# Decayed keys by token: one GpSimd product with a table, two chunks ahead, in place of TensorE transposes and a ScalarE copy

## The chip, the core and the metric

The kernel runs on one core of a Trainium2 chip, as one program. The metric is the device time of one execution in microseconds (us). The engines are named as in the profile: PE (TensorE), PEld (its weight loads), DVE (VectorE), ACT (ScalarE), POOL (GpSimd) and SP (SyncE, which here only starts transfers).

## The reference

Three layers follow each other on 2 sequences of 768 tokens with 384 features. Only the first is touched by the change:

```python
def _attn_ref(r, k, v, w, u):            # B=2, H=8, S=768, D=48
    state = np.zeros((B, H, D, D))
    for t in range(S):
        kt, vt, rt = (k[:, :, t], v[:, :, t], r[:, :, t])
        cur = np.einsum('bhd,bhe->bhde', u[None] * kt, vt)
        y[:, :, t] = np.einsum('bhd,bhde->bhe', rt, state + cur)
        state = w[None, :, :, None] * state + np.einsum('bhd,bhe->bhde', kt, vt)
    return y
```

The second is a mixture of experts: each token takes one of 8 experts by its logits, or that of the token before it, goes through `relu(x @ w1[e]) @ w2[e]`, and is scaled by its probability. The third is a gated MLP with a product across the 768 tokens. Inputs and outputs are float32.

## The kernel before

The attention layer is the first stage of the program and takes about its first 87 us. Its 768 x 2 tokens are cut into 12 chunks of 128 tokens (`NC = 12`), six to a sequence (`NCB = 6`). The loop over tokens becomes products of matrices per chunk, with powers of the decay `w` folded into r and k. All engines run their own list of instructions in order, each in a loop over the chunk number n, and they meet only at semaphores. For one chunk n:

- DVE, `decay(n)` (lines 635 and 636): `k_dec` is k by feature times the table `tab_k`, and `r_dec` is r by feature times `tab_r`. Each is 128 x 512.
- PE, `scores_of(n)` (line 1095): 8 products of `k_dec` and `r_dec`; DVE, `mask(n)` (line 643) keeps the causal half.
- PE, `keysT_of(n)` (line 1108): 4 transposes bring `k_dec` to the layout by token in bank 7. ACT, `keys_of(n)` (line 939) copies that bank to `kn_dec`, two buffers of 128 x 512. There is none for the last chunk of each sequence (n = 5 and 11), so there are 10; `moves(n)` counts them.
- PE, `update(n)` (line 1118): `kn_dec` times v. DVE, `hand_on(n)` (lines 655, 658, 661) adds the old state and decays it for the next chunk.
- PE, `attend(n)` (lines 1134 and 1138): r_dec times the state, and the masked scores times v.
- POOL, `bonus_products(n)` (lines 499 and 502): r times k times u, by token, 128 x 384 each, two chunks ahead of the loop. DVE, `bonus_sum(n)` (line 674) sums it by head. POOL then multiplies v by that sum into `X` (line 514, two instructions; "X products" below), which adds 1 to `s_vc`.
- DVE, `rows_of(n)` (line 667) waits for `attend(n)` and for the X products of n and adds the two into `X`. PE, `rows_transposed(n)` (line 1151) waits for `rows_of(n)` and transposes the rows, ACT copies them (line 945), and PE makes the routing logits from them (`logits_of`, line 1159), which ACT copies out (line 955).

In its loop PE takes scores(n+1), keysT(n+1), attend(n), rows transposed(n-1), update(n+1), logits(n-2). DVE takes mask(n), hand_on(n), decay(n+2), rows_of(n-1), bonus_sum(n+1). POOL takes bonus_products(n+2), the X products of n, and besides: small constants after n = 1 (lines 522 to 552), and after n = 5, 7 and 9 one `make_low` each (line 392), which makes the low half of a piece of expert 0's weights (128 x 1536).

SP loads the inputs in pairs of chunks, double buffered (`load_pair`): rT and kT by feature when `decay` has released the slot, rN and kN by token when `bonus_sum` has, and vN when `attend` and the X products have. All stand in one queue, each behind the one before it.

When all 12 logits are there, DVE works out the routing, which ends with `inv` (line 751). ACT, POOL and PE wait for `inv` before they go on to the experts.

Of the kernel before, what the change touches and what calls it, by code (L numbers as in the profile page):

```python
# [14 lines left out]
P = 128  # L15
# [36 lines left out]
def build(nc, r_feat, k_feat, r_tok, k_tok, v_tok, w_feat, u_tok, w_route, w1, w2, w_in, w_spT, b_sp, w_out, out):  # L52
# [8 lines left out]
    with ExitStack() as ctx:  # L61
        taken = [0]

        def sb(name, shape, dt=F32, scope=ctx):
            size = 2 if dt == BF16 else 4
            for n in shape[1:]:
                size *= n
            taken[0] += -(-size // 32) * 32
            return scope.enter_context(nc.sbuf_tensor(name, shape, dt))

        def sem(name):
            return ctx.enter_context(nc.semaphore(name))
# [85 lines left out]
        xT_att = [sb(f"xT_att{q}", [P, KD, CH], scope=att) for q in range(2)]  # L158
        tab_r = sb("tab_r", [P, NP, CH], scope=att)
        tab_k = sb("tab_k", [P, NP, CH], scope=att)  # L160
        pw = sb("pw", [P, 9, NP], scope=att)
        chunk_decay = sb("chunk_decay", [P, NP, 2 * DH], scope=att)
        state = [sb(f"state{q}", [P, NP, 2 * DH], scope=att) for q in range(2)]
# [86 lines left out]
        s_slot = [sem(f"s_slot{q}") for q in range(2)]  # L250
        s_slot_v = [sem(f"s_slot_v{q}") for q in range(2)]
        s_dec = sem("s_dec")
        s_knT = sem("s_knT")
        s_kn = sem("s_kn")
        s_rk = sem("s_rk")
        s_ruk = sem("s_ruk")
# [141 lines left out]
        def moves(n):  # L398

            return n + 1 - (n + 1) // NCB  # L400
# [3 lines left out]
        @block.sync  # L404
        def _(sp):
            sp.dma_start(pw[:, 0, :], w_feat).then_inc(s_w, 16)

            def load_pair(p):

                slot = p % 2  # L410
                if p >= 2:
                    sp.wait_ge(s_dec, 2 * p - 2)
                for dst, src in ((rT, r_feat), (kT, k_feat)):
                    sp.dma_start(dst[:, slot], src[p]).then_inc(s_slot_f[slot], 16)
                if p >= 2:
                    sp.wait_ge(s_bonus, 2 * p - 2)
                for dst, src in ((rN, r_tok), (kN, k_tok)):
                    sp.dma_start(dst[:, slot], src[p]).then_inc(s_slot[slot], 16)
                if p >= 2:
                    sp.wait_ge(s_y, 2 * p - 2)  # L420
                    sp.wait_ge(s_vc, 2 * p - 2)
                sp.dma_start(vN[:, slot], v_tok[p]).then_inc(s_slot_v[slot], 16)

            load_pair(0)
            sp.dma_start(u_bc[:, :, :].rearrange("p h e -> p (h e)"), u_tok.to_broadcast([P, D])).then_inc(s_small, 16)
            sp.dma_start(w_rt[:, :, :], w_route).then_inc(s_small, 16)
            load_pair(1)
            sp.dma_start(b_bc[:, :], b_sp.to_broadcast([P, S])).then_inc(s_bbc, 16)
            sp.wait_ge(s_const, 1)
            sp.dma_start(x_dram[0:1, :], zero[0:1, :]).then_inc(s_zrow, 16)  # L430
            for p in range(2, NI):
                load_pair(p)

            sp.dma_start(y_dram[E * BLK:, :].rearrange("(i p) d -> p i d", p=P),
                         zero[:, :].rearrange("p (a d) -> p a d", a=1).to_broadcast([P, 2 * NOV, D]))\
                .then_inc(s_zrow, 16)
            for n in range(NRAW, 2 * NRAW):
                load_part(sp, n)

            def store(e, t):  # L440
                sp.wait_ge(s_yev, 2 * e + t + 1)
                sp.dma_start(y_dram[e * BLK + t * P:e * BLK + (t + 1) * P, :], y_out[:, t, :]).then_inc(s_yout[t], 16)

            for e in range(E):
                n = first[e] + 2 * NRAW
                stop = (first[e + 1] if e + 1 < E else n_moe) + 2 * NRAW
                for m in range(n, min(stop, len(parts))):
                    load_part(sp, m)
                for t in range(2):
                    store(e, t)  # L450

            sp.wait_ge(s_meta, 1)
            last = sp.value_load(n_over[0:1, 0:1], min_val=0, max_val=NOV)
            sp.wait_ge(s_low["sp"], 3)
            with sp.If(last >= 1):
                with sp.Fori(1, NOV + 1) as i:
                    with sp.If(i <= last):
                        ex = sp.value_load(ov_e[0:1, bass.ds(i - 1, 1)], min_val=0, max_val=E - 1)
                        for g in range(2):
                            sp.dma_start(raw_as(g, KD), w1_v[bass.ds(ex, 1), :, :, g * FH:(g + 1) * FH]  # L460
                                         .rearrange("a p k f -> p (a k) f")).then_inc(o_raw, 16)
                        for g in range(2):
                            sp.dma_start(raw_as(2 + g, KF // 2),
                                         w2_v[bass.ds(ex, 1), :, g * KF // 2:(g + 1) * KF // 2, :]
                                         .rearrange("a p k n -> p (a k) n")).then_inc(o_raw, 16)
                        for c in range(NC):
                            if c >= 2:
                                sp.wait_ge(o_take, (i - 1) * NC + (c - 1))
                            sp.dma_start(x_in[:, c % 2, :], x_dram[1 + c * P:1 + (c + 1) * P, :]).then_inc(o_x[c % 2], 16)
                        sp.wait_ge(o_yev, i * 2)  # L470
                        for t in range(2):
                            sp.dma_start(y_dram[bass.ds(i * BLK + ((E - 1) * BLK + t * P), P), :], y_out[:, t, :]).then_inc(o_yout, 16)
                        sp.wait_ge(o_yout, i * 32)
                        sp.sem_inc(s_passed_sp, 1)

        @block.gpsimd
        def _(pool):
# [16 lines left out]
            def bonus_products(n):  # L494
# [6 lines left out]
                pool.wait_ge(s_rk, n + 1)  # L501
                nc.gpsimd.tensor_tensor(r_of(n), r_of(n), u_bc[:, :, :], ALU.mult).then_inc(s_ruk, 1)

            bonus_products(0)
            bonus_products(1)
            for n in range(NC):
                p, q = divmod(n, 2)
                if n + 2 < NC:
                    bonus_products(n + 2)
                if q == 0:  # L510
                    pool.wait_ge(s_slot_v[p % 2], 16 * (p // 2 + 1))
# [419 lines left out]

        @block.scalar
        def _(act):
            def keys_of(n):

                act.wait_ge(s_knT, moves(n))
                if moves(n) >= 3:
                    act.wait_ge(s_U, moves(n) - 2)
                nc.scalar.activation(kn_dec[moves(n) % 2][:, :], bank[7][:, :], ACT.Copy).then_inc(s_kn, 1)

            def rowsT_of(n):
                act.wait_ge(s_T, n + 1)
# [11 lines left out]
                act.wait_ge(s_L, n + 1)  # L954
                nc.scalar.activation(logit[:, n, :], bank[7][:, D:D + E + 1], ACT.Copy).then_inc(s_logit, 1)

            keys_of(0)
            for n in range(NC):
                if n + 1 < NC and (n + 2) % NCB:
                    keys_of(n + 1)  # L960
                if n:
                    rowsT_of(n - 1)
                if n >= 2:
                    logit_of(n - 2)
                if n >= 2 and n % 2 == 0:
                    store_rows(n // 2 - 1)
                if n in (1, 3):
                    for m in range(2):
                        load_part(act, n - 1 + m)
                if n in (3, 5, 7, 9):  # L970
                    make_high(act, (n - 3) // 2)
# [106 lines left out]
        def _(pe):  # L1078
# [17 lines left out]
                              k_dec[q][rows, m, :], r_dec[n % 3][rows, m, :], start=True, stop=True)  # L1096
                done.then_inc(s_scores, 1)

            def keysT_of(n):
                pe.wait_ge(s_dec, n + 1)  # L1100
                if n == 3:
                    pe.wait_ge(s_XT, 1)
                if n >= 4:
                    pe.wait_ge(s_logit, n - 3)
                if moves(n) >= 2:
                    pe.wait_ge(s_kn, moves(n) - 1)
                for m in range(NP):
                    done = nc.tensor.transpose(bank[7][:, m * P:(m + 1) * P], k_dec[n % 2][:, m, :], ident[:, :])
                done.then_inc(s_knT, 1)

            def update(n):
                p, q = divmod(n, 2)
                pe.wait_ge(s_slot_v[p % 2], 16 * (p // 2 + 1))
# [28 lines left out]

            def rows_transposed(n):
                pe.wait_ge(s_X, n + 1)
                pe.wait_ge(s_kn, moves(min(n + 2, NC - 1)))
                if n == 1:
                    pe.wait_ge(s_XT, 1)
                if n >= 2:
                    pe.wait_ge(s_logit, n - 1)
                for k in range(KD):  # L1150
                    done = nc.tensor.transpose(bank[7][:, k * P:(k + 1) * P], X[:, n, k * P:(k + 1) * P], ident[:, :])  # L1151
                done.then_inc(s_T, 1)
# [7 lines left out]
                              start=(k == 0), stop=(k == KD - 1))  # L1160
                done.then_inc(s_L, 1)

            keysT_of(0)
            scores_of(0)
            pe.wait_ge(s_small, 32)
            update(0)
            for n in range(NC):
                if n + 1 < NC:
                    scores_of(n + 1)
                    if (n + 2) % NCB:  # L1170
                        keysT_of(n + 1)
                attend(n)
                if n:
                    rows_transposed(n - 1)
                if n + 1 < NC and (n + 2) % NCB:
                    update(n + 1)
                if n >= 2:
                    logits_of(n - 2)
# [221 lines left out]
```

## Time and profile before

| | us |
|---|---|
| median of 3 runs | 406.55 |
| lowest and highest | 405.27, 407.39 |
| the profiled execution, its own time | 407.85 |
| its span in the trace | 406.1 |

Engine busy time over the span, from the page: PE 369.0 us (91%), DVE 203.1 (50%), ACT 141.6 (35%), POOL 189.4 (47%). Busy time of an engine tells how long instructions were running on it; an instruction that shares a resource with another engine's counts for as long as it takes, slowed or not. The 1.75 us between the profiled time and the span lie outside the span. Matmuls overlap each other, so a group's length on PE is best read from the chain of waits, which gives each piece the time until the next begins.

### The profile page before, as it was taken

The numbers are of one execution on the slowest core, as the hardware profiler recorded it, in microseconds if no ns is written. First come the engines' busy times: TensorE is split into PE (matmuls) and PEld (weight loads), VectorE is DVE, ScalarE is ACT, GpSimd is POOL, SyncE is SP. The second block draws the span as 40 slices with busy tenths as digits, with TensorE's granted clock in tenths as the row PEclk, the third lists the DMA queues.
The fourth block names the chain that finished last, engine by engine and source line by source line (L and its number), as shares of the span: only waits on it lengthen the run. The fifth ranks groups of instructions, "written<-read, shape, count | busy, mean of one in ns | idle before, by whom it ended". The sixth has DMA issues, their size and how long they took to land.

```text
span 406.1 us, 6119 instructions
## 1 busy us (share of the span) xinstructions
PE 369.0 (91%) x2481; PEld 348.0 (86%) x2481; DVE 203.1 (50%) x353; ACT 141.6 (35%) x215; POOL 189.4 (47%) x145
## 2 busy tenths in 40 slices
PE   5889999955879998999999999775999999999997
PEld 5789899944669997989899999554999998899996
DVE  7798889426593548562434522124505532803530
ACT  1113223212341656373544505034621224731122
POOL 2796899401948376959586508175500000510000
PEclk9999999975898999999999999998999999999999
DMA  7979979510193958595865810153000011000002
GB/s 266 384 262 382 389 272 363 192 41 0 40 326 111 301 174 310 182 340 177 295 226 163 275 75 2 41 141 93 2 0 0 2 57 62 0 2 0 2 19 97
DMA packets 30671, 61.58 MB, mean 152 GB/s; under 512 B 2417, under 2 KB 17650, under 8 KB 30642
## 3 DMA queue, kind: packets, MB, share of 16 engines
q1 hardware_dynamic: 23634, 47.80, 33.9%
q10 hardware_dynamic: 5216, 7.87, 5.3%
q0 software_dynamic: 1792, 5.51, 4.5%
q8 instruction: 21, 0.34, 0.3%
q14 instruction: 8, 0.07, 0.0%
HBM read 51.33 MB, written 9.83 MB: 151 GB/s over the span
## 4 chain that ended last, share of the span: by engine, by line
PE 66%; DMA 13%; POOL 9%; DVE 4%; issue 3%; ACT 3%; SPq 1%; POOLq 0%; DVEq 0%
PE bank L1204 16%; PE bank L1206 16%; PE bank L1205 16%; POOL w_l L392 8%; DMA x_in<-x_dram,inv 7%; PE bank L1138 4%; PE bank L1095 2%; DMA kT<-k_feat 2%; DMA raw<-w_in 2%; PE bank L1159 2%; PE bank L1134 2%; PE bank L1118 2%; POOL x_in L558 2%; PE bank L1151 1%; DMA y_dram<-y_out 1%
## 5 line engine op out<-in xcount | busy, mean ns | idle before, releaser
L392 POOL TENSOR_TENSOR w_l<-raw,w_h 128x1536 fp32r<-128x1536 f32 x24 | 87.8, 3671 | 34.0 <-ACT w_h L387 33.8
L1204 PE MATMUL bank<-xT_h,w_h 128*128 128x256 f32 x192 | 54.4, 283 | 1.7 <-DVE xT_l L768 1.7
L1205 PE MATMUL bank<-xT_l,w_h 128*128 128x256 f32 x192 | 54.3, 283 | 0.0
L1206 PE MATMUL bank<-xT_h,w_l 128*128 128x256 f32 x192 | 54.3, 283 | 0.0
L387 ACT ACTIVATE w_h<-raw 128x1536 fp32r<-128x1536 f32 x32 | 47.0, 1483 | 18.8 <-DVE inv L751 10.2
L597 POOL TENSOR_TENSOR v_l<-v_nrm,v_h 128x512 fp32r<-128x512 f32 x12 | 15.5, 1291 | 64.4 <-ACT v_h L1051 64.4
L1204 PE MATMUL bank<-w_h,hT_h 128*128 128x384 f32 x128 | 44.0, 344 | 0.0
L1205 PE MATMUL bank<-w_l,hT_h 128*128 128x384 f32 x128 | 43.5, 340 | 0.0
L1206 PE MATMUL bank<-w_h,hT_l 128*128 128x384 f32 x128 | 43.5, 339 | 0.0
L995 ACT ACTIVATE hT_h<-bank 128x512 fp32r<-128x512 f32 x32 | 18.9, 593 | 58.1 <-PE bank L1206 44.4
L1204 PEld LDWEIGHTS bank<-xT_h,w_h 128*128 128x128 f32 x192 | 36.8, 191 | 1.9 <-DVE xT_l L768 1.9
L1206 PEld LDWEIGHTS bank<-xT_h,w_l 128*128 128x128 f32 x192 | 36.8, 192 | 0.0
L1205 PEld LDWEIGHTS bank<-xT_l,w_h 128*128 128x128 f32 x192 | 36.8, 192 | 0.0
L824 DVE SCALAR_TENSOR_TENSOR hT_l<-bank,hT_h 128x512 fp32r<-128x512 f32 x32 | 21.4, 685 | 30.5 <-ACT hT_h L995 23.9
L1206 PE MATMUL bank<-w_sp_h,v_l 128*128 128x384 f32 x96 | 32.1, 334 | 0.0
L1204 PE MATMUL bank<-w_sp_h,v_h 128*128 128x384 f32 x96 | 32.1, 334 | 0.0
L1205 PE MATMUL bank<-w_sp_l,v_h 128*128 128x384 f32 x96 | 32.1, 334 | 0.0
L558 POOL DMA_INDIRECT x_in<-x_dram,inv x16 | 16.8, 1052 | 27.3 <-DVE inv L751 23.8
L1138 PE MATMUL bank<-vN,scores 128*128 128x96 f32 x192 | 28.2, 275 | 0.0
L392 DVE TENSOR_TENSOR w_l<-raw,w_h 128x1536 fp32r<-128x1536 f32 x8 | 23.8, 2977 | 7.0 <-ACT w_h L387 7.0
L777 DVE COPY y_out<-bank 128x384 f32<-128x384 f32 x16 | 8.6, 557 | 36.6 <-PE bank L1206 36.6
L919 DVE TENSOR_TENSOR gate_in<-bank,b_bc 128x384 f32<-128x384 f32 x16 | 8.9, 557 | 35.6 <-PE bank L1206 35.6
(188 smaller groups left out, 842.2 us busy)
## 6 DMA issues: line engine op xcount, KB each, us to landing
raw<-w SPq DMA_DIRECT2D x28, 768.0 KB, 6.3
vN<-v_tok SPq DMA_DIRECT2D x6, 576.0 KB, 5.4
rT<-r_feat SPq DMA_DIRECT2D x6, 512.0 KB, 6.7
kT<-k_feat SPq DMA_DIRECT2D x6, 512.0 KB, 8.1
kN<-k_tok SPq DMA_DIRECT2D x6, 512.0 KB, 7.6
raw<-w ACTq DMA_DIRECT2D x4, 768.0 KB, 10.7
y_dram<-y_out SPq DMA_DIRECT2D x16, 192.0 KB
rN<-r_tok SPq DMA_DIRECT2D x6, 384.0 KB, 5.7
```

Of the source, the lines that this page charges most:

```text
L387: nc.scalar.activation(parts[n][3], raw_of(n), ACT.Copy).then_inc(s_high, 1)
L392: eng.tensor_tensor(low, raw_of(n), high.bitcast(F32), ALU.subtract).then_inc(s_low[kind], 1)
L558: nc.gpsimd.indirect_dma_start(out=x_in[:, t, :], out_offset=None, in_=x_dram, in_offset=bass.IndirectOffsetOnAxis(ap=inv[:, 2 * e + t:2 * ...
L597: nc.gpsimd.tensor_tensor(v_l[:, c, :], v_nrm[q][:, :], v_h[:, c, :].bitcast(F32), ALU.subtract).then_inc(g_vl, 1)
L777: nc.vector.tensor_copy(y_out[:, t, :], bank[4 + t][:, 0:D]).then_inc(s_yev, 1)
L824: nc.vector.scalar_tensor_tensor(hT_l[:, k, :].rearrange("p k t -> p (k t)"), bank[fp][:, :], 0.0, hT_h[:, k, :].rearrange("p k t -> p (k ...
L919: nc.vector.tensor_tensor(gate_in[q][:, :], bank[3 + f][:, 0:HALF], b_bc[:, t * HALF:(t + 1) * HALF], ALU.add).then_inc(g_sin, 1)
L995: nc.scalar.activation(hT_h[:, 2 * fp:2 * fp + 2, :].rearrange("p k t -> p (k t)"), bank[fp][:, :], ACT.Relu).then_inc(s_hh, 1)
L1138: done = mm(bank[4 + q][:, at:at + 2 * DH], scores[q][:, g * NP + m, :], vN[:, p % 2, q, m, g * DH:(g + 2) * DH], start=first_one, stop=Tr ...
L1204: mm(dst, left_h, right_h, start=(k == 0), stop=False)
L1205: mm(dst, left_h, right_l, start=False, stop=False)
L1206: return mm(dst, left_l, right_h, start=False, stop=(k == last_k))
```

## The change

`kn_dec` is no longer made from `k_dec`. k by token (`kN`) is already in SBUF for the bonus. At the start PE transposes the table `tab_k` once, and ACT copies it to a new buffer `tab_kn`. From then on POOL makes `kn_dec` of a chunk as one product `kN * tab_kn` (128 x 512), just ahead of that chunk's bonus products, two chunks ahead of the loop. PE loses the 10 groups of 4 transposes and has the one group of the table; ACT loses 10 copies and has one. `update` waits for POOL's product in place of ACT's copy.

```diff
@@ the load of a pair, SP
                 if p >= 2:
                     sp.wait_ge(s_bonus, 2 * p - 2)
+                    sp.wait_ge(s_kn, moves(2 * p - 3))
                 for dst, src in ((rN, r_tok), (kN, k_tok)):
@@ GpSimd (its wait for s_small stands ahead of this, as before)
+            def keys_of(n):
+                if moves(n) >= 3:
+                    pool.wait_ge(s_U, moves(n) - 2)
+                nc.gpsimd.tensor_tensor(kn_dec[moves(n) % 2][:, :], kN[:, n // 2 % 2, n % 2, :], tab_kn[:, :],
+                                        ALU.mult).then_inc(s_kn, 1)
+
+            pool.wait_ge(s_slot[0], 32)
+            pool.wait_ge(s_tabN, 1)
+            keys_of(0)
             bonus_products(0)
+            keys_of(1)
             bonus_products(1)
             for n in range(NC):
                 p, q = divmod(n, 2)
                 if n + 2 < NC:
+                    if q == 0:
+                        pool.wait_ge(s_slot[(p + 1) % 2], 32 * ((p + 1) // 2 + 1))
+                    if (n + 3) % NCB:
+                        keys_of(n + 2)
                     bonus_products(n + 2)
@@ ScalarE
-            def keys_of(n):
-                act.wait_ge(s_knT, moves(n))
-                if moves(n) >= 3:
-                    act.wait_ge(s_U, moves(n) - 2)
-                nc.scalar.activation(kn_dec[moves(n) % 2][:, :], bank[7][:, :], ACT.Copy).then_inc(s_kn, 1)
+            act.wait_ge(s_tabT, 1)
+            nc.scalar.activation(tab_kn[:, :], bank[7][:, :], ACT.Copy).then_inc(s_tabN, 1)
...
-            keys_of(0)
             for n in range(NC):
-                if n + 1 < NC and (n + 2) % NCB:
-                    keys_of(n + 1)
@@ TensorE
-            def keysT_of(n):
-                pe.wait_ge(s_dec, n + 1)
...
-                for m in range(NP):
-                    done = nc.tensor.transpose(bank[7][:, m * P:(m + 1) * P], k_dec[n % 2][:, m, :], ident[:, :])
-                done.then_inc(s_knT, 1)
-
...
-            keysT_of(0)
+            pe.wait_ge(s_tab, 1)
+            for m in range(NP):
+                done = nc.tensor.transpose(bank[7][:, m * P:(m + 1) * P], tab_k[:, m, :], ident[:, :])
+            done.then_inc(s_tabT, 1)
             scores_of(0)
...
                     scores_of(n + 1)
-                    if (n + 2) % NCB:
-                        keysT_of(n + 1)
                 attend(n)
```

POOL at the start of the attention stage, before: the bonus products of chunks 0, 1 and 2, then the X products of chunk 0.

```order
L499 TENSOR_TENSOR rN<-rN,kN 128x384
L502 TENSOR_TENSOR rN<-rN,u_bc 128x384
L499 TENSOR_TENSOR rN<-rN,kN 128x384
L502 TENSOR_TENSOR rN<-rN,u_bc 128x384
L499 TENSOR_TENSOR rN<-rN,kN 128x384
L502 TENSOR_TENSOR rN<-rN,u_bc 128x384
L514 TENSOR_TENSOR X<-vN,bonus 128x4x48 x2
```

The same place after (line 511 is the new product; 502 and 505 are the bonus products, 532 the X products):

```order
L511 TENSOR_TENSOR kn_dec<-kN,tab_kn 128x512
L502 TENSOR_TENSOR rN<-rN,kN 128x384
L505 TENSOR_TENSOR rN<-rN,u_bc 128x384
L511 TENSOR_TENSOR kn_dec<-kN,tab_kn 128x512
L502 TENSOR_TENSOR rN<-rN,kN 128x384
L505 TENSOR_TENSOR rN<-rN,u_bc 128x384
L511 TENSOR_TENSOR kn_dec<-kN,tab_kn 128x512
L502 TENSOR_TENSOR rN<-rN,kN 128x384
L505 TENSOR_TENSOR rN<-rN,u_bc 128x384
L532 TENSOR_TENSOR X<-vN,bonus 128x4x48 x2
```

Three of the ten products stand ahead of the first X products, and two ahead of the second bonus sum.

POOL from the second `make_low` (`w1_l0`) to the third (`w2_l0`) before: bonus of chunk 10, X of chunk 8, bonus of chunk 11, X of chunk 9.

```order
L392 TENSOR_TENSOR w1_l0<-raw1,w1_h0 128x3x512
L499 TENSOR_TENSOR rN<-rN,kN 128x384
L502 TENSOR_TENSOR rN<-rN,u_bc 128x384
L514 TENSOR_TENSOR X<-vN,bonus 128x4x48 x2
L499 TENSOR_TENSOR rN<-rN,kN 128x384
L502 TENSOR_TENSOR rN<-rN,u_bc 128x384
L514 TENSOR_TENSOR X<-vN,bonus 128x4x48 x2
L392 TENSOR_TENSOR w2_l0<-raw2,w2_h0 128x1536
```

And after:

```order
L394 TENSOR_TENSOR w1_l0<-raw1,w1_h0 128x3x512
L511 TENSOR_TENSOR kn_dec0<-kN,tab_kn 128x512
L502 TENSOR_TENSOR rN<-rN,kN 128x384
L505 TENSOR_TENSOR rN<-rN,u_bc 128x384
L532 TENSOR_TENSOR X<-vN,bonus 128x4x48 x2
L502 TENSOR_TENSOR rN<-rN,kN 128x384
L505 TENSOR_TENSOR rN<-rN,u_bc 128x384
L532 TENSOR_TENSOR X<-vN,bonus 128x4x48 x2
L394 TENSOR_TENSOR w2_l0<-raw2,w2_h0 128x1536
```

The last of the ten products stands here, ahead of the X products of chunk 8; behind it POOL's list is as before.

## Rows read from the trace of the kernel before

**Rows 1.** By stretch: its length; PE, PEld, DVE, ACT, POOL busy; clock, DMA share, GB/s.
```profile
6.00:12.00 6.00, 3.56 (x29) 2.90 (x28) 5.23 (x12) 0.60 (x1) 0.00 (x0) 1.00 0.96 321
...
66.00:72.00 6.00, 6.00 (x63) 5.86 (x61) 5.96 (x10) 1.14 (x4) 5.92 (x5) 1.00 1.05 382
...
84.00:90.00 6.00, 3.17 (x18) 2.19 (x18) 1.60 (x9) 1.13 (x4) 0.00 (x0) 0.72 0.19 68
90.00:96.00 6.00, 1.39 (x7) 1.08 (x7) 4.20 (x17) 0.00 (x0) 0.00 (x0) 0.50 0.00 0
```

**Rows 2.** The chain that ended last: start, us, engine, line, count.
```profile
68.38 0.59 PE bank L1108 x4
...
72.82 0.60 PE bank L1159 x6
...
86.25 1.08 PE bank L1159 x6
```

**Rows 3.** PE by line, 24 to 87.5 us: busy, mean ns, idle before.
```profile
L1151 PE MATMUL bank<-ident,X 128*128 128x128 f32 x36 | 6.0, 276 | 1.9 <-DVE X L667 1.5 <-ACT logit L955 0.4
L1108 PE MATMUL bank<-ident,k_dec 128*128 128x128 f32 x28 | 4.6, 286 | 0.0
```

**Rows 4.** DVE in order of time: start, us, line, operation, [idle before].
```profile
7.82 0.69 DVE L635 TENSOR_TENSOR k_dec<-kT,tab_k 128x512 f32<-128x512 f32 x1
...
18.50 1.27 DVE L643 TENSOR_TENSOR scores<-bank,later 128x512 f32<-128x512 f32 x2
...
20.86 1.48 DVE L635 TENSOR_TENSOR k_dec<-kT,tab_k 128x512 f32<-128x512 f32 x1
...
87.56 0.17 DVE L702 TENSOR_SCALAR take<-logit 128x12 f32<-128x12 f32 x1 [5.12 <-ACT logit L955]
...
98.75 0.17 DVE L751 CAST inv<-bank 128x16 uint32<-128x16 f32 x1 [1.62 <-PE bank L1198]
```

**Rows 5.** ACT: one of the copies of the keys, 69 us.
```profile
69.01 0.60 ACT L939 ACTIVATE kn_dec<-bank 128x512 f32<-128x512 f32 x1 [1.50 <-PE bank L1108]
```

**Rows 6.** POOL in order of time: start, us, line, [idle before].
```profile
12.66 1.00 POOL L499 TENSOR_TENSOR rN<-rN,kN 128x384 f32<-128x384 f32 x1 [9.55 <-DMA w_rt<-w_route]
...
15.78 1.33 POOL L502 TENSOR_TENSOR rN<-rN,u_bc 128x384 f32<-128x384 f32 x1
17.40 1.11 POOL L499 TENSOR_TENSOR rN<-rN,kN 128x384 f32<-128x384 f32 x1 [0.30 <-DMA kN<-k_tok]
...
30.16 0.98 POOL L514 TENSOR_TENSOR X<-vN,bonus 128x192 f32<-128x192 f32 x2
...
38.54 1.44 POOL L499 TENSOR_TENSOR rN<-rN,kN 128x384 f32<-128x384 f32 x1 [3.34 <-DMA kN<-k_tok]
...
46.02 3.45 POOL L392 TENSOR_TENSOR w_l<-raw,w_h 128x1536 fp32r<-128x1536 f32 x1
...
64.17 1.43 POOL L514 TENSOR_TENSOR X<-vN,bonus 128x192 f32<-128x192 f32 x2
...
75.08 0.97 POOL L514 TENSOR_TENSOR X<-vN,bonus 128x192 f32<-128x192 f32 x2 [0.64 <-DVE bonus L674]
```

**Rows 7.** POOL by line, 12.6 to 76.1 us: busy, mean ns, idle before.
```profile
L502 POOL TENSOR_TENSOR rN<-rN,u_bc 128x384 f32<-128x384 f32 x12 | 13.8, 1153 | 0.9
L499 POOL TENSOR_TENSOR rN<-rN,kN 128x384 f32<-128x384 f32 x12 | 13.2, 1096 | 14.6 <-DMA w_rt<-w_route 9.5 <-DMA kN<-k_tok 5.1
```

**Rows 8.** SP's issues of the token-layout loads: start, us.
```profile
29.51 0.52 SPq L418 DMA_DIRECT2D kN<-k_tok x1
...
59.32 0.33 SPq L422 DMA_DIRECT2D vN<-v_tok x1
```

**Rows 9.** PE in order of time: start, us, line, operation.
```profile
35.97 0.49 PE L1151 MATMUL bank<-ident,X 128*128 128x128 f32 x3
...
71.46 0.49 PE L1151 MATMUL bank<-ident,X 128*128 128x128 f32 x3
...
81.69 0.49 PE L1151 MATMUL bank<-ident,X 128*128 128x128 f32 x3
```

More of the change, by code:

```diff
@@ L160, in build @@
         tab_k = sb("tab_k", [P, NP, CH], scope=att)
+        tab_kn = sb("tab_kn", [P, H * DP], scope=att)
         pw = sb("pw", [P, 9, NP], scope=att)
@@ L252, in build @@
         s_dec = sem("s_dec")
-        s_knT = sem("s_knT")
+        s_tabT = sem("s_tabT")
+        s_tabN = sem("s_tabN")
         s_kn = sem("s_kn")
@@ L1097, in scores_of @@
                 done.then_inc(s_scores, 1)
-            def keysT_of(n):
-                pe.wait_ge(s_dec, n + 1)
[L1101 to L1106, printed above, removed]
-                for m in range(NP):
-                    done = nc.tensor.transpose(bank[7][:, m * P:(m + 1) * P], k_dec[n % 2][:, m, :], ident[:, :])
-                done.then_inc(s_knT, 1)
             def update(n):
@@ L1144, in rows_transposed @@
                 pe.wait_ge(s_X, n + 1)
-                pe.wait_ge(s_kn, moves(min(n + 2, NC - 1)))
+                if n == 0:
+                    pe.wait_ge(s_tabN, 1)
                 if n == 1:
```

## The prediction, made before the changed kernel ran

> **What bounds the kernel now.** I read the table of stretches first, then the chain of waits, then each engine's instructions in order of time, and last POOL's groups by line.
>
> The change lies in the attention stage. In the stretch from 66 to 72 us PE is busy 6.00 of 6 us, but DVE is at 5.96 and POOL at 5.92 as well [rows 1]. The chain of waits runs through PE to the last logits at 86.25 [rows 2]. PE hardly stands idle in it: ahead of its transposes of rows 1.9 us in all, of which 1.5 once for `rows_of` [rows 3]. So PE bounds the stage, and two engines follow it closely. The question is what PE waits for once it has less to do.
>
> Behind the logits the routing begins at 87.56 and ends in `inv` at 98.75 [rows 4]. ACT, POOL and PE all wait for `inv`, and what follows in their lists is unchanged, so I take the rest of the program to move with the end of the attention stage, microsecond for microsecond.
>
> **What is removed.** PE loses its ten groups of 4 transposes of keys and has one for the table. Seven of the ten lie in the stretch that PE bounds (28 instructions, [rows 3]). One takes 0.59 us on the chain [rows 2], so 7 x 0.59 = 4.1 us, if nothing else becomes late. The three earlier ones lie ahead of 24 us, where transfers and DVE lead; I count them as nothing. ACT loses ten copies of 0.60 us; ahead of the one shown it had idled 1.50 us [rows 5], so it bounds nothing, and this is worth nothing. That the keys are ready two chunks ahead takes away no wait either: the update with them never ends an idle time of PE after 24 us.
>
> **What is added: the price of one product.** The trace has no two-input product of 128 x 512 on POOL, so I bound it. One of 384 columns takes 1.00 us when nothing disturbs it, one of 1536 columns 3.45 us [rows 6]. The slope is 2.45 / 1152 = 2.13 ns per column, so 512 columns cost 1.00 + 128 x 0.00213 = 1.27 us undisturbed. The lower bound is 1.00 us, that of the smaller product. Disturbed, the smaller ones take up to 1.33 [rows 6], a third more (a single one with its start behind a transfer 1.44), which gives 1.69 us as the upper bound. On average the 24 bonus products take (1.096 + 1.153) / 2 = 1.12 us [rows 7], 12% over 1.00. I take the same 12% for the new one: 1.43 us.
>
> The disturbance is mutual. DVE's `k_dec` takes 0.69 us while POOL is idle and 1.48 while POOL is in its products [rows 4]. The Trainium skill's page "GPSIMD Engine Reference", section "Key points", says that GpSimd shares its SBUF interfaces with VectorE and contends with VectorE instructions that have two SBUF inputs; `decay` is such an instruction, and the trace agrees. By that rule a product that met `decay` all along would cost the upper bound, one that never met it the undisturbed price. The same page's section "Engine selection" gives elementwise work on a tile to VectorE; by it this change loads the wrong engine, though DVE, at 5.96 of 6, has no room here either.
>
> **What lies in POOL's way.** From its first product at 12.66 to the end of the X products of chunk 8 at 64.17 + 1.43 = 65.60 POOL takes 52.94 us. Of that it idles 5.1 us for kN [rows 6, 7]. With the gaps between its instructions it is thus at work for 47.84 us. All ten new products stand ahead of this point, as the order shows. With them: 47.84 + 10 x 1.43 = 62.1 us.
>
> Do the waits for kN remain? POOL would come to the keys of chunk 6 at 38.54 - 3.34 - 0.30 + 5 x 1.43 = 42.1. Their kN was issued at 29.51 and was there at 38.54 [rows 6, 8]; if the issue moves by 2 us, as the bonus sum that releases it does (below), it is there at 40.5, still in time. So the idle 5.1 us are used up, and the sum has already given that credit. X of chunk 8 ends at 12.66 + 62.1 = 74.8 us in place of 65.60.
>
> **When it is needed.** `rows_of(8)` follows it at once and takes 0.5 us, and PE's transposes of those rows follow that, at about 74.8 + 0.55 = 75.35. Before, they started at 71.46 [rows 9]. The shift is 75.35 - 71.46 = +3.9 us.
>
> From there on no engine's list differs from before: the last transposes of keys were at 68.38 [rows 2]. POOL's next deadlines are met. X of chunk 9 is two bonus products and one pair later, at about 78; its rows are transposed some 5.7 us behind those of chunk 8. The third `make_low` (3.45 us undisturbed) and X of chunks 10 and 11 end near 84, before at 75.08 + 0.97 = 76.05 [rows 6]; chunk 10's transposes were at 81.69 [rows 9] and come at 85.6. So the tail from 71.46 to 87.56, 16.1 us, stays, and the stage ends 3.9 us later.
>
> **The same working earlier.** At the start two new products stand ahead of the second bonus sum, behind which `mask(1)` is queued on DVE. That bonus product ended at 15.78 + 1.33 = 17.11 [rows 6] and now ends 1.27 + 1.43 later at 19.8, so `mask(1)`, at 18.50 before [rows 4], starts near 20.3: +1.8 us. Five new products stand ahead of X of chunk 2: 30.16 + 0.98 - 0.30 + 7.15 = 38.0, its rows are transposed at 38.55 in place of 35.97 [rows 6, 9]: +2.6 us. Up to chunk 8 PE then sheds five groups, 2.95 us, and would come there 0.35 us early. PE's gain is really taken, and waited away: it stands still for some 4 us for X of chunk 8.
>
> **Waits added or moved.** SP's new wait for `s_kn` comes after that for `s_bonus`, and POOL makes the bonus product after the keys, so it costs nothing. vN is released by X products: the last went out at 59.32 [rows 8] and would now wait for X of chunk 7, about 9 us (a `make_low`, a key, two bonus and two X products) ahead of 74.8, so at 65.6. Moved 6 us later, it is used 10 us later, by the update of chunk 10 at 76; behind it in SP's queue stand only weight loads for after `inv`. The copy and transposes of the table (0.60 + 0.59 us behind the table, which is ready where `k_dec` starts, 7.82 [rows 4]) end near 9.3, ahead of POOL's start at 12.66, and are hidden. The first update now waits for the first product, 1.3 us, inside the +1.8.
>
> **Sum.** +3.9 us. The profiled execution took 407.85 us, so it would take 411.75. The median of the runs shown is 406.55, 1.3 us under that; against it I predict 406.55 + 3.9 = 410.5.
>
> With the price k of one product the shift is 10 k - 10.4: +6.5 us at 1.69, +2.3 at 1.27, -0.4 at 1.00. A tenth of a microsecond on the product is a microsecond on the kernel.
>
> **The rivals.** A measurement of this kernel can tell about 0.5%, 2.0 us, from no change. That is reached at k = 1.24.
>
> - *Hidden, no change.* k between 1.00 and 1.24: POOL is late, but by no more than PE has gained. Shift -0.4 to +2.0, about 407.5. For it: the bound of 1.00. Against it: POOL's two sizes give 1.27 undisturbed, and DVE is in the way.
> - *PE's gain stays (the other side).* With POOL not in the way, the end moves by 1.8 for the late start less 4.1: -2.3, or 404.2. It decides if X of chunk 8 ends before about 70.5, so if k is under 1.0, or if POOL's work holds hidden waits that go. For it: PE is busy 6.00 of 6 [rows 1]. Against it: 5.1 us of idle time must take in ten products of at least 1 us.
> - *The clock.* PE gets stalls of 2 to 4 us. The granted clock fell to a mean of 0.72 in 84 to 90 us and was 0.50 (1.2 GHz of 2.4) in 90 to 96, with PE busy 1.39 us [rows 1]; a group of logits took 1.08 us there in place of 0.60 [rows 2]. If it fell at chunk 8, most of the 16.1 us behind would be PE work at half speed: 7 us more, about 418. Against it: with 3.56 us busy in 6 to 12 us the clock stayed at 1.00.
>
> **How the numbers follow.** The forecast (k from 1.24 to 1.69, 408.6 to 413) 0.69; hidden 0.16; PE's gain 0.09; the clock 0.06. Slower by over 0.5%: 0.69 + 0.06 = 0.75; within: 0.16; faster: 0.09. The range goes from 405.3, which leaves out most of the faster case, to 414.3: that is 1.3 us above the upper bound, for DVE's own products, which the added ones can slow from 0.69 to 1.48. It leaves out the clock. The likeliest case's own range is 408.6 to 413.
>
> **What would show it.** Right: POOL busy with hardly a gap from 12.7 to about 84 us; the new product at 1.3 to 1.7 us; PE idle ahead of its transposes of rows, released by DVE's X, near 36 to 38 and for about 4 us near 71 to 75; DVE waiting there for X products; `inv` at about 102.7. Wrong: idle time of POOL in the stage, a product near 1.0 us, PE waiting in the update for `kn_dec` rather than for rows, or `inv` late by 4 us and the end not.

## The result and the profile after

The changed kernel is slower. Its median is 411.91 us (410.98 to 422.19, 5 runs) against 406.55 us (405.27 to 408.05, 5 runs); the ratio is 1.0135, with a 95% interval of 1.0091 to 1.0178. In a second set, that of the first experiments, it was 414.67 us against 404.52: ratio 1.0241 (1.0197 to 1.0286). Sets differ (the last three ran on three different chips): the kernel before has medians of 406.55, 404.52, 409.39 and 410.41 us in the four sets here. So each experiment is read by the kernel before of its own set, and, finer, by landmarks in its trace.

Ratios and their intervals leave out executions over 1.5% above the fastest of the same kernel (here 422.19 and 418.07 us), so a ratio can differ from that of the medians. The only profile of the changed kernel in the first set is of the execution of 422.19 us, with a mean granted clock of 0.926; the profile read below is therefore one from the second set, of 415.27 us (span 413.5).

The landmark is `inv`, the end of attention and routing, at 98.75 us before [rows 4]. In the changed kernel, DVE in order of time:

```profile
98.86 0.17 DVE L720 TENSOR_SCALAR take<-logit 128x12 f32<-128x12 f32 x1 [5.14 <-ACT logit L969]
...
110.04 0.17 DVE L769 CAST inv<-bank 128x16 uint32<-128x16 f32 x1 [1.62 <-PE bank L1199]
```

The stage ends 11.3 us later, not 3.9 (9.3 against the second profile of the kernel before, where `inv` is at 100.74). GpSimd, by line, from 12 to 90 us (busy, mean ns, idle before):

```profile
L502 POOL TENSOR_TENSOR rN<-rN,kN 128x384 f32<-128x384 f32 x12 | 14.4, 1200 | 0.0
L505 POOL TENSOR_TENSOR rN<-rN,u_bc 128x384 f32<-128x384 f32 x12 | 13.9, 1162 | 0.9
L511 POOL TENSOR_TENSOR kn_dec<-kN,tab_kn 128x512 f32<-128x512 f32 x10 | 13.8, 1380 | 9.6 <-DMA w_rt<-w_route 9.2 <-PE bank L1117 0.4
```

The new product takes 1.38 us on average, and GpSimd no longer waits for kN. POOL in order of time, around the X products of chunks 7 and 8:

```profile
64.92 1.42 POOL L532 TENSOR_TENSOR X<-vN,bonus 128x192 f32<-128x192 f32 x2
...
66.31 3.46 POOL L394 TENSOR_TENSOR w_l<-raw,w_h 128x1536 fp32r<-128x1536 f32 x1
...
74.07 0.97 POOL L532 TENSOR_TENSOR X<-vN,bonus 128x192 f32<-128x192 f32 x2
```

X of chunk 8 ends at 75.04 us. TensorE's transposes of rows, for chunks 2, 3, 7 and 8 (before: 35.97 for chunk 2, 71.46 for chunk 8, [rows 9]):

```profile
39.62 0.73 PE L1151 MATMUL bank<-ident,X 128*128 128x128 f32 x3 [2.61 <-DVE X L685]
48.58 0.49 PE L1151 MATMUL bank<-ident,X 128*128 128x128 f32 x3
...
73.78 0.75 PE L1151 MATMUL bank<-ident,X 128*128 128x128 f32 x3 [1.79 <-DVE X L685]
82.73 0.49 PE L1151 MATMUL bank<-ident,X 128*128 128x128 f32 x3
```

TensorE waits 2.61 us for chunk 2's rows and 1.79 for chunk 7's, and does not wait for chunk 8's. But the distance from 2 to 3 is 8.96 us and from 7 to 8 it is 8.95. In the kernel before, chunks 3 and 7 stood here, 5.73 us behind chunk 2 and 6.18 ahead of chunk 8:

```profile
41.70 0.49 PE L1151 MATMUL bank<-ident,X 128*128 128x128 f32 x3
...
65.28 0.55 PE L1151 MATMUL bank<-ident,X 128*128 128x128 f32 x3
```

The stretches of the changed kernel say why (columns as in [rows 1]):

```profile
12.00:20.00 8.00, 6.30 (x38) 5.94 (x39) 3.85 (x5) 0.00 (x0) 7.55 (x7) 0.57 1.02 414
...
40.00:46.00 6.00, 6.00 (x36) 5.75 (x35) 5.14 (x7) 2.15 (x3) 5.92 (x7) 0.50 0.53 184
66.00:72.00 6.00, 5.95 (x57) 5.64 (x57) 5.97 (x7) 2.04 (x3) 6.00 (x4) 1.00 0.77 241
74.00:80.00 6.00, 6.00 (x37) 5.75 (x35) 5.13 (x9) 0.67 (x2) 5.92 (x8) 0.50 1.02 381
```

Behind each of the three stalls (3.37 us ahead of the first update, 2.61, 1.79) the granted clock is 0.50, the 1.2 GHz level (the first stretch, at a mean of 0.57, starts inside the stall). The first profile of the kernel before has 1.00 in all these places. And the chain of waits, which ran through PE before [rows 2], now has this piece (start, us, what):

```profile
56.13 1.26 DVE k_dec L653
57.51 1.49 DVE r_dec L654
...
64.03 1.48 DVE r_dec L654
65.51 0.47 DVE X L685
65.98 0.46 DVE bonus L692
66.44 1.20 DVE scores L661 x2
67.63 0.47 DVE state_sum L676
...
71.78 1.47 DVE r_dec L654
73.25 0.48 DVE X L685
73.78 0.75 PE bank L1151 x3
```

The wait of 2.61 us for chunk 2 is GpSimd's: VectorE stood idle 2.96 us for the X products, which ended at 38.90. The wait of 1.79 us for chunk 7 is VectorE's: the X products had ended at 66.34, and `rows_of(7)` at 73.72. From 56 to 74 us VectorE's own list is the bound: its instructions follow each other without a gap, and those with two SBUF inputs are slow (the gaps in the chain are the product of the state and `k_dec`, told as "issue" there). In order of time the worst is the state's product, under GpSimd's `make_low` of 66.31 to 69.77:

```profile
68.13 2.05 DVE L679 TENSOR_TENSOR state<-state_sum,chunk_decay 128x384 f32<-128x384 f32 x1
70.10 1.75 DVE L653 TENSOR_TENSOR k_dec<-kT,tab_k 128x512 f32<-128x512 f32 x1
```

By line, 12 to 88 us, before:

```profile
L636 DVE TENSOR_TENSOR r_dec<-rT,tab_r 128x512 f32<-128x512 f32 x10 | 11.8, 1182 | 0.0
L661 DVE TENSOR_TENSOR state<-state_sum,chunk_decay 128x384 f32<-128x384 f32 x8 | 6.0, 747 | 0.3
```

and after:

```profile
L654 DVE TENSOR_TENSOR r_dec<-rT,tab_r 128x512 f32<-128x512 f32 x10 | 13.6, 1361 | 0.0
L679 DVE TENSOR_TENSOR state<-state_sum,chunk_decay 128x384 f32<-128x384 f32 x8 | 8.1, 1016 | 0.3
```

### The profile page after: what moved, and what is told of

It is laid out like the page before. It is cut to its first block, busy times and chain, and to the rows that moved or that the text cites. A ratio compares the mean times of both kernels' runs of the same rounds, so it can differ in the third digit from the quotient of the medians.

```text
span 420.4 us, 6040 instructions
## 1 busy us (share of the span) xinstructions
PE 382.6 (91%) x2445; PEld 360.4 (86%) x2445; DVE 203.5 (48%) x353; ACT 136.1 (32%) x206; POOL 203.3 (48%) x155
## 4 chain that ended last, share of the span: by engine, by line
PE 57%; POOL 18%; DMA 11%; DVE 5%; issue 4%; ACT 3%; SPq 1%; POOLq 0%; DVEq 0%
PE bank L1205 15%; PE bank L1207 15%; PE bank L1206 15%; POOL w_l L394 7%; DMA x_in<-x_dram,inv 5%; PE bank L1137 3%; POOL XG L606 3%; PE bank L1159 2%; DMA w_rt<-w_route 2%; PE bank L1133 2%; DMA raw<-w_out 2%; PE bank L1106 2%; POOL kn_dec L511 2%; DMA raw<-w_in 2%; POOL x_in L576 2%
## 5 line engine op out<-in xcount | busy, mean ns | idle before, releaser
L394 POOL TENSOR_TENSOR w_l<-raw,w_h 128x1536 fp32r<-128x1536 f32 x24 | 86.7, 3625 | 34.2 <-ACT w_h L389 34.0
L389 ACT ACTIVATE w_h<-raw 128x1536 fp32r<-128x1536 f32 x32 | 47.0, 1484 | 20.1 <-DVE inv L769 10.2
L1137 PE MATMUL bank<-vN,scores 128*128 128x96 f32 x192 | 34.6, 318 | 0.0
L1137 PEld LDWEIGHTS bank<-vN,scores 128*128 128x128 f32 x192 | 31.0, 233 | 0.3 <-issue 0.2
L959 ACT ACTIVATE xT_att<-bank 128x384 f32<-128x384 f32 x12 | 5.9, 491 | 68.0 <-PE bank L1151 68.0
```

The lines of the kernel that those rows point to most:

```text
L389: nc.scalar.activation(parts[n][3], raw_of(n), ACT.Copy).then_inc(s_high, 1)
L394: eng.tensor_tensor(low, raw_of(n), high.bitcast(F32), ALU.subtract).then_inc(s_low[kind], 1)
L1137: done = mm(bank[4 + q][:, at:at + 2 * DH], scores[q][:, g * NP + m, :], vN[:, p % 2, q, m, g * DH:(g + 2) * DH], start=first_one, stop=Tr ...
```

## The experiments

The changed kernel again, with no edit:

> The changed kernel once more, for a profile of an execution at the time of its median. Queue theory (GpSimd's list is too long, X products of chunk 8 come too late): 411 to 412.5 us; X of chunk 8 ends near 75 us with GpSimd idle under 1 us from 12.6 on, TensorE waits about 3 to 4 us ahead of the transposed rows of chunk 8. Clock theory (the stall at the start, 3.7 us ahead of the first update, lets the granted clock fall, and that is the loss): same total time, but the stretch 12 to 24 us at a clock well under 1.00, and TensorE not waiting for X of chunk 8.

414.67 us, `inv` at 110.04. X of chunk 8 at 75.04 and GpSimd's idle time of 0.4 us are as the queue theory says; the wait for chunk 8 that it names is not there. Each theory is half right, and the one that VectorE bounds was in neither.

**Ten products that nobody reads, in the kernel before.**

```diff
+            def spare_of(n):
+                if moves(n) >= 3:
+                    pool.wait_ge(s_spare, moves(n) - 2)
+                nc.gpsimd.tensor_tensor(kn_spare[moves(n) % 2][:, :], kN[:, n // 2 % 2, n % 2, :],
+                                        tab_k[:, :, :].rearrange("p m t -> p (m t)"), ALU.mult).then_inc(s_spare, 1)
@@ at the places of keys_of in the changed kernel
+                        spare_of(n + 2)
```

> The kernel before, with ten extra GpSimd products of 128x512 at the places where the changed kernel has its ten, into a buffer that nobody reads; TensorE keeps its transposes and ScalarE its copies. Queue theory: the ten products are the cost and the relief of TensorE is waited away, so the time is that of the changed kernel or a little above: 411 to 413.5 us. Rival (the loss comes from the first update waiting for GpSimd, and from the clock after it): this kernel's first update does not wait, so under 408.5 us.

414.01 us, ratio 1.0219 (1.0166 to 1.0272), beside 1.0241 for the changed kernel on the same chip; `inv` at 107.40. The first update waits 0.24 us here. So the whole loss comes with the ten products, and taking the transposes and copies away gives nothing back that can be measured. One product takes 1.433 us.

The way to the loss is not the same here. TensorE waits 2.12 us for chunk 2's rows, as in the changed kernel, and the granted clock has a mean of 0.55 in 40 to 46 us and 0.60 in 46 to 52, so that chunk 3's rows come 10.15 us behind chunk 2's:

```profile
39.79 0.55 PE L1169 MATMUL bank<-ident,X 128*128 128x128 f32 x3 [2.12 <-DVE X L685]
49.94 0.85 PE L1169 MATMUL bank<-ident,X 128*128 128x128 f32 x3
...
60.00:72.00 12.00, 12.00 (x123) 11.71 (x122) 11.20 (x17) 4.50 (x8) 11.92 (x10) 1.00 0.74 245
```

From 54 to 86 us TensorE, which keeps its transposes, is busy all the time at a clock of 1.00, and VectorE is not the bound. Of the 8.65 us by which `inv` is later than in the first profile of the kernel before, 3.8 are there at chunk 2's rows and 8.2 at chunk 3's: GpSimd's queue and the half clock behind its stall make this loss.

**The three make_low behind the last X products, in the changed kernel.**

```diff
-                if n in (5, 7, 9):
-                    make_low(pool, (n - 5) // 2)
@@ after the loop
+            for n in range(3):
+                make_low(pool, n)
```

> The changed kernel with GpSimd's three make_low of the attention stage (10.3 us) moved behind its last X products. Queue theory: two of them, 7 us, lie ahead of X of chunk 8, which then ends near 68 and is no longer waited for; what is left is the late start (+1.8) less the transposes (-4.1): 403.5 to 406 us. Clock theory: the start is unchanged, so 410 to 412.5 us.

409.66 us median of 12 (403.7 to 412.18); the ratio is 1.0009 (0.997 to 1.0048), that of the plain medians 1.013: five of its times lie from 403.7 to 406.7 us, one at 409.15, six from 410.16 to 412.18. What spreads them stays open. `inv` is at 106.28, 3.8 us earlier than in the changed kernel, and the state's product takes 1.15 us where it took 2.05. With that, chunk 7's rows come 1.0 us earlier (72.76), and TensorE's stall ahead of them is 0.63 us in place of 1.79; the clock stays at 1.00, and chunk 8's rows follow after 5.79 us in place of 8.95. Most of the 3.8 us is thus the clock. That nothing changes, as the clock theory had it, is refuted. The queue theory's number is met by four of its times, but not in the stage: X of chunk 8 ends at 73.07 in place of the 68 expected, and VectorE is busy 11.97 of 12 us from 62 to 74, as before the edit.

**Matmuls that nobody reads at the start of the changed kernel.**

```diff
             scores_of(0)
+            idle_work(12)      # 12 x mm(bank[6][:, 384:512], ident, ident)
             pe.wait_ge(s_small, 32)
```

> The changed kernel with 12 matmuls of 128x128 whose result nobody reads between the first scores and the first update, in the time in which TensorE waits for the first GpSimd product. Queue theory: 411 to 412.5 us, as without them. Clock theory: the clock stays at 1.00 from 12 to 24 us and the time falls by 2 to 5 us, to 407 to 410; there are also fewer executions near 418 to 422.

416.43 us, ratio 1.0301 (1.0255 to 1.0346); `inv` is at 107.39, 2.7 us earlier, in a profile of the fastest of six executions (411.36 us). The stall ahead of the first update is 0.49 us in place of 3.37, but the clock then fell later, to a mean of 0.81 in 24 to 36 us and, behind a stall of 3.04 us for chunk 5's rows, 0.75 in 60 to 72. The start alone is not the cause.

**X products first.** GpSimd's loop takes the X products of n, then keys and bonus of n + 2:

```diff
                 p, q = divmod(n, 2)
-                if n + 2 < NC:
...
-                        keys_of(n + 2)
-                    bonus_products(n + 2)
                 if q == 0:
                     pool.wait_ge(s_slot_v[p % 2], 16 * (p // 2 + 1))
...
                 done.then_inc(s_vc, 1)
+                if n + 2 < NC:
...
+                        keys_of(n + 2)
+                    bonus_products(n + 2)
```

> The changed kernel with GpSimd's order turned round in its loop: the X products of chunk n first, then the keys and bonus of chunk n+2. So far the changed kernel is at 1.024 of the kernel before (414.7 us), the kernel before with ten idle products at 1.022. Queue theory (X products late behind the keys): each X product comes some 3.5 us earlier, TensorE's stall near 36 to 40 us, where chunk 2's row waited for it, goes, and the ratio falls to 1.005 to 1.012. Contention theory (the added products slow VectorE's own products, and VectorE's list gets too long): GpSimd does as much as before beside VectorE, so the ratio stays at 1.018 to 1.026.

416.17 us against 409.39, ratio 1.0238 (1.0162 to 1.0314). X of chunk 8 ends 3.9 us earlier, at 71.12, and chunk 2's rows are transposed at 36.89 with no wait. `inv` comes to 105.52, 4.5 us earlier, 3.2 of it because chunk 8's rows follow chunk 7's (72.19) after 5.78 us; the clock did not fall there. The ratio is in the contention theory's band, but that of the plain medians is 1.017, and in this set the kernel before against itself gives 1.0069 (below), so the total does not decide between the two theories. VectorE now waits for bonus products (4.2 us), and its state product takes 1.24 us on average.

**Ten memsets in place of the ten idle products.**

```diff
-                nc.gpsimd.tensor_tensor(kn_spare[...][:, :], kN[...], tab_k[...], ALU.mult).then_inc(s_spare, 1)
+                nc.gpsimd.memset(kn_spare[moves(n) % 2][:, :], 0.0).then_inc(s_spare, 1)      # 1344 columns
```

> The kernel before, with ten GpSimd memsets of 1344 columns (1.2 to 1.3 us each by the smaller ones) in place of the ten idle products: the same time in GpSimd's queue, but no reads beside VectorE's. Queue theory: the time is that of before_ten, ratio 1.018 to 1.026. Contention theory: VectorE's k_dec, r_dec and state products are no slower than in the kernel before (1.09, 1.18, 0.75 us) and the ratio is 1.000 to 1.008.

412.7 us against 409.39, ratio 1.0128 (1.0066 to 1.0191; plain medians 1.008): between the two. A memset takes 1.22 us. X of chunk 8 ends at 71.13, the rows of chunk 8 start at 74.88 against 71.46 and 73.11 in the two profiles of the kernel before, and `inv` is at 102.58. The clock stayed at 1.00 from 24 to 84 us.

A memset does not slow VectorE's products. Three `r_dec` lie wholly beside one (at 16.52, 41.04 and 67.48 us), and each takes 0.68 us; the longest product, a `k_dec` of 3.93 us, lies beside a `make_low`:

```profile
40.59 1.22 POOL L511 MEMSET kn_spare<- 128x1344 f32 x1 [0.49 <-DMA kN<-k_tok]
41.04 0.68 DVE L653 TENSOR_TENSOR r_dec<-rT,tab_r 128x512 f32<-128x512 f32 x1
...
63.26 3.75 POOL L394 TENSOR_TENSOR w_l<-raw,w_h 128x1536 fp32r<-128x1536 f32 x1
63.63 3.93 DVE L652 TENSOR_TENSOR k_dec<-kT,tab_k 128x512 f32<-128x512 f32 x1
```

That one makes the mean of `k_dec` 1.39 us; the other nine have 1.10, and `r_dec` has 0.94. So this run has the longer GpSimd queue nearly without the added contention, and it ends 1.8 to 3.8 us behind the kernel before by `inv`, where the ten products cost 6.7 to 8.7. What the ten products cost beyond that is not one thing: a product is 0.2 us longer, it slows VectorE, and X of chunk 2 ends 1.9 us later than here (39.07 against 37.13), with a stall of 2.12 us in place of 0.77 and the half clock behind it. The run does not split these.

**TensorE's stalls filled, in the changed kernel.**

```diff
+            idle_work(15)      # ahead of the first update
@@ loop
                 attend(n)
+                for _ in range({3: 18, 6: 4, 7: 4, 8: 12}.get(n, 0)):
+                    mm(bank[2 * (n % 2)][:, 0:P], ident[:, :], ident[:, :], start=True, stop=True)
                 if n:
                     rows_transposed(n - 1)
```

> The changed kernel with matmuls that nobody reads in TensorE's stalls: 15 ahead of the first update, 18 ahead of the transposed rows of chunk 2, 4, 4 and 12 ahead of those of chunks 5, 6 and 7. Stalls alone: the time stays at ratio 1.022 to 1.028. Clock as amplifier (each stall is followed by some 6 to 7 us at half the clock, which costs about 3 us again): clock near 1.00 up to 84 us, and the ratio falls to 1.005 to 1.013.

417.98 us against 409.39, ratio 1.0263 (1.0191 to 1.0334; plain medians 1.021): the time did not fall. The stretches show that the edit did what it should:

```profile
12.00:20.00 8.00, 7.92 (x81) 7.34 (x80) 3.57 (x5) 0.00 (x0) 7.47 (x7) 1.00 1.03 412
40.00:46.00 6.00, 6.00 (x62) 5.86 (x61) 4.90 (x7) 2.15 (x3) 5.84 (x8) 1.00 0.48 164
74.00:80.00 6.00, 6.00 (x62) 5.86 (x61) 5.97 (x10) 0.67 (x2) 5.92 (x8) 1.00 1.01 380
```

and TensorE's rows of chunks 2, 7 and 8:

```profile
41.10 0.49 PE L1156 MATMUL bank<-ident,X 128*128 128x128 f32 x3
...
73.75 0.55 PE L1156 MATMUL bank<-ident,X 128*128 128x128 f32 x3
79.54 0.49 PE L1156 MATMUL bank<-ident,X 128*128 128x128 f32 x3
```

The filling itself makes chunk 2's rows 1.5 us later. At full clock chunk 3's are 1.5 us earlier all the same (47.06), but chunk 7's come at 73.75, the same as 73.78 at changing clock: VectorE sets that time (its state product took 2.94 us at 67.20, under a `make_low`). Chunk 8's follow 5.79 us later in place of 8.95, and `inv` is at 107.83 in place of 110.04. That is what the half clock costs this stage, 2 to 3 us. The total does not show it; the later stages took 308.1 us here against 303.5 in the profile of the changed kernel, which is of another chip.

**The kernel before, once more.**

> The kernel before once more, for a second profile. The first shows one stall of TensorE of 4.3 us with no releaser at the start of the last layer, which no profile of a changed kernel has. If it is a chance of that one execution, the span here is 400 to 403 us without it; if it belongs to the kernel before, it is here too and the time is 404 to 408 us.

410.23 us; against the kernel before of its own set the ratio is 1.0069 (1.0023 to 1.0115), for the same code. Differences of that size are thus not to be read from these ratios, and those of this set (1.0238, 1.0128, 1.0263) may be high by as much. The stall is there again (4.1 us), so it is not of one execution; `inv` is at 100.74.

**r_dec by a ScalarE copy, in the changed kernel.**

```diff
-                nc.vector.tensor_tensor(r_dec[n % 3][:, :, :], rT[:, p % 2, q], tab_r[:, :, :], ALU.mult)
@@ ScalarE, two chunks ahead
+                nc.scalar.activation(r_dec[n % 3][:, :, :], rT[:, p % 2, q], ACT.Copy).then_inc(s_rd, 1)
```

> The changed kernel with r_dec made by a ScalarE copy instead of VectorE's product (it leaves out r's decay factor, so other tokens go to other experts and the later stages can take another time: only the time of inv, the end of the attention stage and the routing, is compared; it is 110.0 us in the changed kernel, 98.8 and 100.7 in two profiles of the kernel before). VectorE is without its 1.36 us product in each chunk. VectorE's list bounds (GpSimd's added products slow it until it has no idle time): TensorE's wait for the rows of chunk 7 near 73.8 goes and inv is at 101 to 104 us. GpSimd's queue bounds: the X products come as late as before and inv stays above 106 us.

The run leaves out the decay factor of r. `inv` at 105.07: between the two numbers, and nearer to the queue's. VectorE now has room and waits for X products, 5.1 us in three waits, 4.19 of them for chunk 2; chunk 7's rows still come at 72.14, with a state product of 2.42 us under GpSimd's `make_low` ahead of them. With VectorE relieved, GpSimd's lateness takes its place. Of the 5.0 us gained by `inv`, 1.6 are there at chunk 7's rows; 3.2 come behind them, where the clock did not fall.

**Half the columns in the new product.**

```diff
-                nc.gpsimd.tensor_tensor(kn_dec[...][:, :], kN[...], tab_kn[:, :], ALU.mult)
+                nc.gpsimd.tensor_tensor(kn_dec[...][:, 0:256], kN[..., 0:256], tab_kn[:, 0:256], ALU.mult)
```

> The changed kernel with the GpSimd product over 256 of the 512 columns (it leaves out half of the keys by token, so again only inv is compared). The prediction said that the kernel's time follows ten times the product's price: the price falls from 1.38 to some 0.75 us, 6.3 us in all. If that slope holds until TensorE bounds again, inv is at 103 to 105 us; if TensorE's relief then counts, as low as 97 to 100.

The run leaves out half of the keys by token. The product takes 0.896 us, 0.48 less. X of chunk 8 ends at 72.03, 3.0 us earlier, not 4.8, since GpSimd now waits again (2.4 us for the update, 0.7 for kN). `inv` at 103.63, inside the first band: halving the product gives 6.4 us back, 3.0 of it at chunk 7's rows (70.76) and 3.2 behind them, where the clock did not fall. TensorE's relief of 4.1 us shows nowhere: `inv` stays 2.9 to 4.9 us behind the kernel before.

**Both repairs, and the control.** The changed kernel with the X products first and the make_low behind:

> The changed kernel with both edits: the X products of chunk n ahead of the keys of n+2, and the three make_low behind the last X products. If GpSimd's length and order are what hurts: inv at 99 to 103 us, and the time within 0.5% of the kernel before on the same chip, or faster. If VectorE stays the bound through its slowed products: inv above 104.

412.44 us against 410.41, ratio 1.0006 (0.9969 to 1.0043; plain medians 1.005); `inv` at 101.61, the earliest of the changed kernels, in a profile of the fastest of its twelve executions (407.39 us; one took 470.68). With GpSimd free of its late work the change costs nothing that the total can tell, and wins nothing; the stage is still 2.5 us longer than in the control below.

> The kernel before with only the three make_low moved behind the last X products, as the control of that edit. TensorE bounds that stage in the kernel before, so nothing is expected of the stage: inv at 98 to 100 us, time within 0.5% of the kernel before. If the make_low also slow VectorE's products enough to matter, inv is 1 to 3 us earlier.

410.82 us, ratio 0.9977 (0.9939 to 1.0016); `inv` at 99.09. No version here beats the kernel before.

## Why the prediction came out as it did

The direction was right: +3.9 us was forecast, +5.4 us was measured in the first set, +10.2 in the second. That the size fits is luck in good part. The ratio of the second set, put on 406.55 us, is 416.3, above the range that ends at 414.3. And the stage that the sum is about ended 9.3 to 11.3 us later, with `inv` at 110.04 where about 102.7 was expected. The way there was right in part.

- *The price of the product.* 1.43 us was taken, 1.38 measured (1.433 for the idle one in the kernel before). Interpolating between GpSimd's two sizes and adding the average disturbance of its neighbours held.
- *GpSimd's queue.* X of chunk 8 was put at 74.8 us and ended at 75.04; that of chunk 2 at 38.0 against 38.90, and its rows at 38.55 against 39.62. The credit of 5.1 us for kN was right as well.
- *"PE's transposes of those rows follow that, at about 75.35."* This is the step that failed. They started at 82.73, and at 79.54 with the clock held at 1.00. TensorE stood still for chunk 2, as forecast (2.61 us), but then for chunk 7 (1.79 us) in place of some 4 us for chunk 8, each time with the half clock behind it. The step took VectorE's list as having nothing else to do. Beside the added products VectorE's products with two SBUF inputs are slower (`r_dec` 1.36 us against 1.18 and 1.16 in the two profiles of the kernel before, `k_dec` 1.21 against 1.09 and 0.95, state 1.02 against 0.75 and 0.88), and an engine that was busy 5.96 of 6 us [rows 1] had no room for that; chunk 7's rows were late for it, 7.4 us behind its X products. The row that said so, 0.69 against 1.48 us [rows 4], was used for GpSimd's price and for 1.3 us of the range, not for VectorE's list. It is not the whole of the loss: with TensorE's transposes kept, VectorE is not the bound, and the half clock behind chunk 2's stall makes 4.4 of the 8.65 us (ten products that nobody reads, above).
- *"The tail stays."* From chunk 8's rows to `inv` it took 27.29 us before and 27.31 after. That held.
- *The clock.* Given 0.06 as a case that goes to 418. In the trace it is no separate case: it follows each stall, in three places, and costs the stage 2 to 3 us. In the execution of 422.19 us it was at 0.50 from 42 to 60 us, behind a stall of 2.62 us for chunk 2, and `inv` came at 117.42: 7.4 us more, though not at the place that the case names. The evidence against it, 3.56 us busy in 6 us at a clock of 1.00, was a single stretch with a shorter stall.
- *"The rest moves with the end of the attention stage."* Not shown. From `inv` to the end the span is 307.4 and 307.7 us in two profiles of the kernel before, 303.5 in the changed one of the second set, and between 301.1 and 310.0 over all profiles. A part is a wait of TensorE at the start of the last layer, of 0.8 to 5.7 us. It goes more with the set, and so perhaps with the chip, than with the edit (301.1 to 303.5 in the four profiles of the second set, 306.8 to 309.3 in the four of the third), but what sets it was not tried and stays open. Whether the stage's loss in the first set was larger than the +5.4 us is not shown, since its only profile of the changed kernel is that of 422.19 us; the total agrees with the forecast closer than the parts do.

The half-columns run measured the slope: 13 us of `inv` per microsecond of product in place of the 10 of the sum; half of that, 3.2 of 6.4 us, is one fall of the clock that went away. By the sum, 10 k - 10.4, the change would win 1.4 us at 0.896 us; the stage still ended 2.9 to 4.9 us later than before.

## What to carry to other kernels

Before work goes to an engine that looks half idle over the span, read its busy share in the stage at hand, and that of every engine whose instructions share a resource with it: an engine at 5.96 of 6 us that is slowed becomes the bound, although nothing was added to its list. Such a meeting has no average price: a long GpSimd product can hold a VectorE product for its whole length (3.9 us in three runs) or not at all. Taking work off the engine that bounds a stage pays only if what comes next has slack; here 4.1 us came off and none of it could be found in the result. A short new stall of TensorE has to be priced with the clock behind it.

## What the runs showed of the hardware

- A VectorE product with two SBUF inputs that starts while a GpSimd product of 128 x 1536 runs does not go slower in proportion; it ends when the GpSimd product has ended, and a little more. In all 23 such cases of the profiles here (`k_dec`, `r_dec` or state product under a `make_low`) the end is 0.41 to 0.55 us behind that of the `make_low`, whether the product took 0.56 us or 3.98. In the changed kernel the state product of 68.13 us, above, ends at 70.18, 0.41 behind the `make_low` of 66.31 to 69.77. So the cost hangs on how the two meet: in the two profiles of the kernel before, with the same three `make_low`, none of these products took over 1.50 us.
- Beside the smaller GpSimd products VectorE's products of 512 columns go from 0.69 to 0.99 or 1.48 us. A GpSimd memset does not hold them: 0.68 us beside one.
- Stalls of 3.37, 2.61 and 1.79 us were followed by the 1.2 GHz level. In the kernel before stalls of 1.72 and 1.51 us were not, but its version with the late make_low had a mean of 0.86 in 12 to 24 us behind one of 1.79 us. One of 1.78 us that ended near 21.8 us was followed by a mean of 0.64 in 20 to 26 us with the matmuls at the start, and by 1.00 with the stalls filled. So stalls of that length can go either way. Useless matmuls in the stalls kept the clock at 1.00 from 12 to 88 us.
- The same program took medians from 404.5 to 410.4 us on three chips, and the kernel before measured twice gave a ratio of 1.0069 within one set.
